# Splitting w1 and w2 on two engines, with transposes and value products at earlier steps

## The reference, cut to what matters

```python
def _attn_ref(q, k, v):                      # (4, 8, 576, 64) each, float32
    scores = (1 / sqrt(64)) * q @ k.T        # per batch and head
    mask = (rel >= 0) & (rel < 64)           # rel = query position - key position
    attn = softmax(where(mask, scores, -1e9))
    return attn @ v

def reference(...):
    x = attention, rows = 4 * 576 = 2304 tokens, 8 heads * 64 = 512 columns
    a = x @ w1; b = x @ w2                   # 512 x 1024 each
    x = (a * b @ w3) @ w_out                 # 1024 x 1024, 1024 x 512
    # then 8 experts, one for each token by argmax(x @ w_gate)
    h = maximum(x[mask] @ ew1[e], 0)         # 512 x 1024
    out[mask] = gate * sigmoid(x @ w_output_gate)[e] * (h @ ew2[e])
```

## Time and profile before

| | us |
|---|---|
| time, median of 3 runs | 707.28 (707.17 to 707.4) |
| the profiled execution | 707.28, with a span of 705.2 |
| TensorE busy | 697.6, 99% of the span |
| DVE, ACT, POOL busy | 368.5, 267.6, 106.0 |
| granted TensorE clock | 1.00 of full speed throughout |

### The profile page before, as it was taken

One profiled execution on the slowest core, in us unless ns is written; L12 is line 12 of the kernel. 1 busy time (PEld: TensorE's weight loads), 2 busy tenths in 40 slices (PEclk: granted clock), 3 DMA queues, 4 the chain that ended last, 5 costly groups with the idle time before them and its releaser, 6 DMA issues.

```text
span 705.2 us, 14721 instructions
## 1 busy us (share of the span) xinstructions
PE 697.6 (99%) x5075; PEld 636.5 (90%) x5076; DVE 368.5 (52%) x693; ACT 267.6 (38%) x651; POOL 106.0 (15%) x173
## 2 busy tenths in 40 slices
PE   8999999999999999999999999999999999999997
PEld 6999999999999999999999999888888888888885
DVE  5488566346444634634563568845456444652211
ACT  4365433243234223324322254444465534542221
POOL 7110000100100100010000001222222222222211
PEclk9999999999999999999999999999999999999999
DMA  9674202311320231140017044745356644411110
GB/s 330 244 251 165 75 27 72 117 44 59 99 68 27 78 115 49 49 136 31 4 58 269 2 167 145 281 150 171 125 188 213 226 149 161 162 35 45 33 45 30
DMA packets 29485, 82.73 MB, mean 117 GB/s; under 512 B 3645, under 2 KB 3645, under 8 KB 29440
## 3 DMA queue, kind: packets, MB, share of 16 engines
q1 hardware_dynamic: 24400, 66.63, 28.4%
q0 software_dynamic: 5040, 15.47, 6.4%
HBM read 72.65 MB, written 10.49 MB: 118 GB/s over the span
## 4 chain that ended last, share of the span: by engine, by line
PE 98%; DMA 1%; ACT 0%; POOLq 0%; SPq 0%; issue 0%; ACTq 0%
PE bank L476 29%; PE bank L478 28%; PE bank L477 27%; PE bank L592 3%; PE bank L568 3%; PE bank L749 3%; PE bank L727 1%; PE bank L580 1%; DMA w3r<-in_w3T 1%; PE bank L489 1%; PE bank L709 1%; PE bank L506 0%; PE bank L504 0%; PE bank L502 0%; PE bank L519 0%; PE bank L525 0%
## 5 line engine op out<-in xcount | busy, mean ns | idle before, releaser
L476 PE MATMUL bank<-Wh,abh 128*128 128x272 f32 (+1 forms) x288 | 84.3, 293 | 0.0
L478 PE MATMUL bank<-Wh,abl 128*128 128x272 f32 (+1 forms) x288 | 82.0, 285 | 0.0
L1103 DVE TENSOR_TENSOR wbuf<-raw,wbuf 128x1024 f32 (+1 forms) x64 | 75.3, 1220 | 12.5 <-ACT wbuf L874 12.4
L477 PE MATMUL bank<-Wl,abh 128*128 128x272 f32 (+1 forms) x288 | 81.7, 284 | 0.0
L1302 DVE TENSOR_TENSOR hTl<-bank,hTh 128x512 fp32r<-128x512 f32 x44 | 28.4, 685 | 96.9 <-ACT hTh L922 96.9
L1124 DVE TENSOR_TENSOR ab_f<-bank,a_sb 128x384 f32<-128x384 f32 x48 | 26.7, 557 | 93.7 <-PE bank L478 92.8
L476 PE MATMUL bank<-wbuf,hTh 128*128 (+1 forms) x176 | 70.7, 402 | 0.0
L476 PE MATMUL bank<-wbuf,xsTh 128*128 (+1 forms) x176 | 70.4, 400 | 0.0
L478 PE MATMUL bank<-wbuf,hTl 128*128 (+1 forms) x176 | 68.8, 391 | 0.0
L478 PE MATMUL bank<-wbuf,xsTl 128*128 (+1 forms) x176 | 68.6, 390 | 0.0
L477 PE MATMUL bank<-wbuf,xsTh 128*128 (+1 forms) x176 | 68.6, 390 | 0.0
(11 more groups left out here) (215 smaller groups left out, 1458.4 us busy)
## 6 DMA issues: line engine op xcount, KB each, us to landing
raw<-in_expert_w SPq DMA_DIRECT2D x64, 512.0 KB, 4.5
qk<-in_qk SPq DMA_DIRECT2D x24, 448.0 KB, 4.0
vv<-in_v SPq DMA_DIRECT2D x24, 384.0 KB, 3.3
x_rows<-x_sb POOLq DMA_DIRECT2D x18, 256.0 KB, 3.1
w3r<-in_w3T SPq DMA_DIRECT2D x8, 512.0 KB, 3.7
wo<-in_w_out SPq DMA_DIRECT2D x8, 256.0 KB, 8.8
woT<-in_w_outT SPq DMA_DIRECT2D x4, 512.0 KB, 8.8
w1r<-in_w SPq DMA_DIRECT2D x4, 512.0 KB, 4.4
```

Of the source, the lines that this page charges most:

```text
L476: pe.matmul(dst, lh, rh, start=first, stop=False)
L477: pe.matmul(dst, lh, rl, start=False, stop=False)
L478: return pe.matmul(dst, ll, rh, start=False, stop=last)
L1103: dve.tensor_tensor(wbuf[:, bass.ds(wcol(e, part, 1, c * PC), PC)], raw[part * NP1 + c][:, :], f32(wbuf[:, bass.ds(wcol(e, part, 0, c * PC ...
```

## The change

The names of the six tables stay, and `turned` and `valued` get other steps, in the fold and in all chunks alike. In the fold, w2 is loaded and split ahead of w1; the eight splits stand at eight steps, one each; the low halves of parts 0, 1, 3 and 5 are made by POOL, behind the `normal` of the same step; `weigh` moves from the front of `own` to its end, behind W's low half; SP's loads are ordered anew. In the first hidden tile of chunk 0 TensorE waits for two counters, one of POOL's and one of DVE's low halves. Another semaphore gets a new name and keeps its use.

```diff
-        w12 = [(w1h, w1l, w1r, w1, kt) for kt in range(KD)] + [(w2h, w2l, w2r, w2, kt) for kt in range(KD)]
+        w12 = [(w2h, w2l, w2r, w2, kt) for kt in range(KD)] + [(w1h, w1l, w1r, w1, kt) for kt in range(KD)]
...
         def turned(e):
-            return {4: 0, 7: 1, 9: 2, 11: 3}.get(e)
+            return {3: 0, 6: 1, 9: 2, 11: 3}.get(e)
 
         def valued(e):
-            return {7: 0, 9: 1, 11: 2}.get(e)
+            return {5: 0, 8: 1, 11: 2}.get(e)
...
-        w12_steps = {4: (0,), 6: (1,), 7: (2,), 11: (3,), 13: (4,), 14: (5,), 15: (6, 7)}
+        w12_steps = [4, 6, 8, 10, 11, 12, 13, 14]
+        w12_pool = (0, 1, 3, 5)
+        pool_count = lambda n: sum(i in w12_pool for i in range(n))
...
-                if i < KD:
+                if i >= KD:
                     sp.wait_ge(wo_lo, KF)
...
             load_v(0)
+            load_w12(0)
             load_v(1)
             load_qk(2)
-            load_w12(0)
+            load_w12(1)
             load_qk(3)
             load_w3(4)
-            load_w12(1)
             load_w3(6)
             load_w12(2)
             load_w3(5)
-            load_qk(4)
             load_w12(3)
             load_w12(4)
+            load_qk(4)
+            load_w12(5)
+            load_v(2)
             load_w3(7)
-            load_v(2)
+            load_w12(6)
             load_qk(5)
-            load_w12(5)
-            load_w12(6)
             load_w12(7)
...
-                            if cc == 0 and f == 0:
-                                pe.wait_ge(w12_lo, m * KD + kt + 1)
+                            if cc == 0 and f == 0 and m == 0:
+                                pe.wait_ge(w12_lo_pool, pool_count(KD + kt + 1))
+                                pe.wait_ge(w12_lo_dve, KD + kt + 1 - pool_count(KD + kt + 1))
...
                 def own():
-                    if weighed(i - 2) is not None:
-                        weigh(0, weighed(i - 2))
                     if i - 1 in w3_steps:
                         lo_w3(w3_steps[i - 1])
...
                     dve.tensor_tensor(Wl[:, ws], w_bank(i)[:, 0:end - first], f32(Wh[:, ws]), ALU.subtract).then_inc(W_lo, 1)
+                    if weighed(i - 2) is not None:
+                        weigh(0, weighed(i - 2))
...
-            normalise(0)
+            def lo_w12(i):
+                wh, wl, wr, _, kt = w12[i]
+                ws = slice(kt * FF, (kt + 1) * FF)
+                pool.wait_ge(w12_hi, i + 1)
+                pool.tensor_tensor(wl[:, ws], wr[:, ws], f32(wh[:, ws]), ALU.subtract).then_inc(w12_lo_pool, 1)
+
+            for i in range(len(w_order)):
+                if weighed(i - 2) is not None:
+                    normal(0, weighed(i - 2))
+                if i in w12_steps and w12_steps.index(i) in w12_pool:
+                    lo_w12(w12_steps.index(i))
```

More of the change, by code:

```diff
@@ L225, in build @@
         W_done, W_hi, W_lo = sem("W_done"), sem("W_hi"), sem("W_lo")
-        w12_hi, w12_lo = sem("w12_hi"), sem("w12_lo")
+        w12_hi, w12_lo_pool, w12_lo_dve = sem("w12_hi"), sem("w12_lo_pool"), sem("w12_lo_dve")
         qk_in, v_in = [sem(f"qk_in{i}") for i in range(2)], [sem(f"v_in{i}") for i in range(2)]
@@ L243, in build @@
         raw_in = [sem(f"raw_in{c}") for c in range(2 * NP1)]
-        ew_hi, ew_lo = [sem("ew1_hi"), sem("ew2_hi")], [sem("ew1_lo"), sem("ew2_lo")]
+        ew_hi, ew_lo = [sem("ew1_hi"), sem("ew2_hi")], [sem("ew12_lo_dve"), sem("ew2_lo")]
         idx_ok, tab_ok, scale_ok = sem("idx_ok"), sem("tab_ok"), sem("scale_ok")
@@ L329, in build @@
         w3_steps = {1: 3, 5: 4, 7: 5, 9: 6, 11: 7}
-        w12_steps = {4: (0,), 6: (1,), 7: (2,), 11: (3,), 13: (4,), 14: (5,), 15: (6, 7)}
+        w12_steps = [4, 6, 8, 10, 11, 12, 13, 14]
+        w12_pool = (0, 1, 3, 5)
+        pool_count = lambda n: sum(i in w12_pool for i in range(n))
+        assert len(w12_steps) == 2 * KD
         def wo_piece(n, i):
@@ L867, in _ @@
                     exps(0, raised(i - 2))
-                for part in w12_steps.get(i, ()):
-                    hi_w12(part)
+                if i in w12_steps:
+                    hi_w12(w12_steps.index(i))
             def split_hi(e, part, c):
@@ L1039, in lo_w12 @@
                 dve.wait_ge(w12_hi, i + 1)
-                dve.tensor_tensor(wl[:, ws], wr[:, ws], f32(wh[:, ws]), ALU.subtract).then_inc(w12_lo, 1)
+                dve.tensor_tensor(wl[:, ws], wr[:, ws], f32(wh[:, ws]), ALU.subtract).then_inc(w12_lo_dve, 1)
             def weight_splits(i):
-                for part in w12_steps.get(i, ()):
-                    lo_w12(part)
+                if i in w12_steps and w12_steps.index(i) not in w12_pool:
+                    lo_w12(w12_steps.index(i))
             def wo_lo_out(j, lo, hi, full):
```

## The result

| | us |
|---|---|
| time before, beside it on the same chip | 707.34, median of 6 runs (707.17 to 708.09) |
| time after | 712.68, median of 6 runs (710.63 to 714.25) |
| ratio | 1.0073, with an interval of 1.0056 to 1.0088 |
| the profiled execution after | 712.73, with a span of 711.0 and a mean granted clock of 0.996 |

The change makes the kernel slower by 5.3 us. The forecast was 709.9 with a range of 708.0 to 712.5: the direction came true, the size did not, and the time lies just above the range. The forecast was +2.6 us, so the question is where the 2.8 us between 709.9 and 712.68 came from.

A forecast was written before the change was run, and what follows sets the result against it. TensorE's matmul stream, 98% of the chain, was taken to bound the kernel. 707.28 us plus 1.4 for the borders of split groups and 1.2 for the wait for the reciprocal gave 709.9 us, with a range of 708.0 to 712.5.

The forecast's parts named there:

- The bound: Whole kernel: TensorE is 98% of the chain, with at most 0.25 us of idle time to win in the fold.
- the two ways named: On TensorE: a change of order can alter the matmul stream's own cost or bring in a new wait.
- The borders: Attention groups split on TensorE in the fold and five chunks: 0.23 us in each of six stages, +1.4 us.
- the small terms: Extra per split group on TensorE: t, v, s 0.21 us; t, s 0.01; t, v 0.01.
- dear transposes: Rival for t alone on TensorE: it costs 0.53 us, giving 713.3 us; chance 0.08.
- cheap transposes: Rival for t alone on TensorE: it hides under large matmuls, down to 705.1 us; chance 0.06.
- The wait: Fold, step 13: TensorE's t of piece 3 waits once for POOL's `normal`, +1.2 us, bounds 0 and 2.1.
- DVE's low half of that part can start when its 1.05 us is over: Fold, step 12: DVE starts on w1's part at about 62.4, once ACT's 1.05 us and 0.1 signal are over.
- exps begins where it did, at 59.22: Fold, ACT: exps keeps its start, because the value product it waited for now lies a step back.
- What I cost at nothing: POOL's four low halves, w2 ahead of w1, new loads, two counters and piece 0's earlier turn: no cost.
- a longer stall: Rival in the fold: `normal` takes 1.73 us or a POOL low half blocks it; 710.8, up to 712; chance 0.13.
- The 2.1 us around it stay: Outside the span: the 2.1 us between span and profiled time were taken as unchanged.

The follow-up runs named there:

- x3_tables_only: The kernel before with the new `turned` and `valued` steps alone; 709.2 us, ratio 1.0025.
- x1_weigh_front: The changed kernel with `weigh` back at the front of `own` in the fold; 709.45 us, ratio 1.0028.
- x6_one_low_half_back: The changed kernel with the low half of part 3 (step 10) back on DVE, the other three still on POOL; 710.58 us, ratio 1.0042.
- x2_old_tables: The changed kernel with `turned` and `valued` as before; 708.83 us, ratio 1.0017.
- x4_weigh_only: The kernel before with `weigh` at the end of `own` in the fold and nothing else; 709.49 us, ratio 1.0025.
- x10_front_and_old: The changed kernel with `weigh` at the front and the old `turned` and `valued`, all else kept; 707.08 us, ratio 1.0000.
- x0_change_again: The changed kernel run once more, unchanged; 712.62 us, ratio 1.0071.
- x7_filled_wait: The changed kernel with 12 matmuls that nothing reads on TensorE ahead of the t of step 13; 711.63 us, ratio 1.0055.
- x9_long_wait: The kernel before with `weigh` at the end of `own` and two DVE memsets ahead of the `weigh` of step 12; 711.5 us, ratio 1.0057.
- x8_merged_groups: The kernel before with chunk groups rejoined, t alone at three tiles, v and s together at two, fold unchanged; 706.5 us, ratio 0.9992.
- x11_best_of_both: The changed kernel with `weigh` at the front, all low halves on DVE, old tables in the fold, joined groups in chunks; 708.13 us, ratio 1.0008.

## Why the prediction was right or wrong

**The bound: right.** TensorE's stream sets the end, and the change acted by the two ways named: what the stream costs, and a new wait. The views were the right ones.

**The borders: right, 1.7 us for 1.4.** A t alone costs 0.33 to 0.36 us in the chunks of after, for the 0.34 worked out from four transposes. Timeline of PE behind tile 3 of chunk 0, of after:

```profile
94.50 0.34 PE L481 MATMUL bank<-xTh,w2l 128*128 128x384 f32 x1
94.67 0.49 PE L583 MATMUL bank<-ident,prob 128*128 128x128 f32 x3
94.92 0.42 PE L479 MATMUL bank<-xTh,w1h 128*128 128x384 f32 x1
95.18 0.33 PE L480 MATMUL bank<-xTl,w1h 128*128 128x384 f32 x1
```

No gap ahead (0.17), 0.25 of body, 0.26 for 0.17 behind. The v alone costs 1.05, as taken over from s. What was short are the small terms. Read over the matmuls of the tile behind each group, t and s side by side cost 1.35 and apart 0.35 + 1.04 = 1.39, 0.04 more and not 0.01; t, v and s 2.18 and apart 0.35 + 1.05 + 1.03 = 2.43, 0.25 more and not 0.21; t and v 1.38 and apart 1.40, 0.02 more and not 0.01. That is 0.31, for 0.30 from chunk to chunk; a chunk has 60.52 us where 60.4 was forecast. `x3_tables_only` shows the whole term by itself, 1.7 us. The rivals *dear transposes* and *cheap transposes* both fall with these rows.

**The wait: the mechanism right, its size wrong, 2.48 us for 1.2.** The place, the engine and the cause were as forecast, and undoing that one edit gives back most of the loss (`x1_weigh_front`). The step that failed is "DVE's low half of that part can start when its 1.05 us is over": DVE was not free then, and ACT was late too, as "exps begins where it did, at 59.22" failed for the same reason. It rests on the paragraph *What I cost at nothing*, which asked of POOL's low halves only whether they hold up POOL's own `normal`, and not what they do to DVE. The terms: ACT's part 0.25 later than reckoned (`exps` began at 59.46, behind DVE), DVE 0.48 late to take it (its maximum was 1.72 longer), 0.13 more from the low half to rec, which gives rec at 64.92 for 64.05; 0.14 from `normal`'s end to the t, a signal that the sum had left out; and TensorE wants the t 0.26 earlier, 0.21 of it because its stream began sooner. 0.87 + 0.14 + 0.26 = 1.27, and 1.2 + 1.27 = 2.47.

It stood in the text already that `normal` takes 1.73 beside a DVE operation with two SBUF inputs and 0.83 without, and that the four low halves would slow what DVE does of this kind. That was made into a rival (*a longer stall*) with `normal` as its victim, and the sum went on without it. `normal` was undisturbed (0.83, as taken); what was slowed was on the other engine, and 8 us ahead of rec. By the rows this operation accounts for 0.25 + 0.48 of the 1.27; `x6_one_low_half_back`, where the t is 1.90 late, shows that it does so at all; the share of the new steps of t and v (2.48 for 1.85) came to light by `x2_old_tables`, and of these steps the sum had taken only that TensorE comes later and that a wait of ACT goes.

**The clock: not in the sum at all, 1.5 us.** Neither the sum nor a rival had it, since the trace of before shows 1.00 throughout and no wait of this length. With a wait of 1.2 us, as forecast, it would have been no mistake: `x4_weigh_only` and two others show no drop behind waits of 1.33 to 1.73. It is a cost that comes with the error of size, 1.52 on top of 1.27, and the time left the range by the two together. The range reached 712.5 for a longer stall and for a part of dear transposes; neither had a clock in it.

**The time around the span: held to stay, 0.35 less.** "The 2.1 us around it stay" did not come true (1.73 in after). The sum would be further from the time measured without this, so in this term the errors cancel by luck.

**What was costed at nothing: right by itself, wrong beside the other two edits.** `x10_front_and_old` has all of it and is at 1.0000. The loads, w2 ahead of w1, the two counters and piece 0's earlier turn in a chunk brought no wait.

**How well the account holds.** For each kernel the sum of borders (1.7, or -0.6 for joined groups), lateness (for `x11_best_of_both` with its v at step 15), clock (1.52 where it fell) and -0.34 for low halves on POOL, against the difference of the medians:

| kernel | sum, us | measured, us |
|---|---|---|
| after | 5.36 | 5.34 |
| x0_change_again | 5.36 | 5.38 |
| x1_weigh_front | 2.0 | 1.94 |
| x2_old_tables | 1.5 | 1.32 |
| x3_tables_only | 1.7 | 1.69 |
| x4_weigh_only | 1.5 | 1.98 |
| x6_one_low_half_back | 3.3 | 3.34 |
| x7_filled_wait | 3.8 | 4.39 |
| x9_long_wait | 4.2 | 4.26 |
| x10_front_and_old | -0.2 | -0.37 |
| x8_merged_groups | -0.6 | -0.95 |
| x11_best_of_both | 0.4 | 0.68 |

`x4_weigh_only` and `x7_filled_wait` stand about 0.5 us above their sums; the others are within 0.35. In the first the profiled execution (708.62) is 0.9 below the median, so its trace can't show the rest; in the second the fold's first t already stands 0.76 later than in after (35.78 for 35.02), ahead of anything that was edited. The terms are read from the same kernels' traces, so the table says that they add up, not that they would forecast another kernel.

## What to carry to other kernels

An operation handed to POOL isn't free because POOL is idle: look at what DVE does meanwhile, take every DVE operation there with two SBUF inputs as lasting until POOL's is over, and follow that engine's queue to the next thing that TensorE waits for. A small instruction on which another engine waits belongs ahead of the large ones of its step, not behind them. And a new wait of TensorE has two prices, its length and, if it gets long, the matmuls behind it at half the clock: here waits of up to 1.73 us cost their length alone, and those of 2.32 and 2.50 cost 1.5 us more, so a wait shorter by 0.6 gave back 2.0 us in `x6_one_low_half_back`.

## What the runs showed of the hardware

- **POOL holds DVE up, and the other way round, nearly to the end of the operation.** DVE's maximum of 128x384 has two inputs in SBUF. It takes 0.56 us alone, and 2.28, 1.84 and 2.75 beside POOL's low half (the last in after, at 34.30), which itself stays at 2.39 or 2.40; each time it ends 0.41 or 0.42 behind POOL's (in `x2_old_tables` 55.95 + 1.84 = 57.79 against 54.98 + 2.40 = 57.38). Where DVE was first, POOL was late, and so in turn: in `x1_weigh_front` `normal` takes 1.72 for 0.83 behind DVE's w3 low half (61.75 to 62.95), DVE's next low half 1.85 for 1.22 behind `normal`, and POOL's low half 3.38 for 2.39 behind that. The Trainium skill (SBUF — State Buffer, section Who interferes with whom) calls the port pair of the two an exclusive lock and says that the order of issue, not the shape, decides who blocks. The trace agrees with it: in each of these pairs the later one is slowed. DVE's operations with one input in PSUM are not: the pair of operations of `masks` that reads the scores (L998) takes 1.01 beside a low half on POOL (44.45 in after) and 1.01 without (54.43 in before).
- **The granted clock** was 0.50 for some 3.5 us behind waits of 2.32 and 2.50 us (as the view of the waits has them) and 1.00 behind those of 1.33, 1.69 and 1.73. Matmuls of 256 columns then stand 0.21 apart instead of 0.12. The Trainium skill (TensorE: Matmul & The Clock Gate, section What's actually happening) has the same two levels and none between them, which the two spacings bear out; a stretch that shows 0.78 or 0.86 is a mixture of both.
- **Borders in a stream of large matmuls.** A group of 24 matmuls with 64 rows takes 0.09 us on entering and 0.11 on leaving beside its body; three transposes with all 128 rows take nothing on entering (94.50 to 94.67 in after) and 0.09 on leaving. Two groups of 64 rows side by side save 0.2 us (1.87 for 1.05 and 1.03 in `x8_merged_groups`). That the number of rows makes the difference is not tested.
